# Dividing in two instructions per step in a fused DFT and two-layer kernel on one Trainium2 core

## What is computed

```python
X = np.fft.fft(np.fft.fft(x, axis=1), axis=2).real      # x: (2, 3008, 256)
h = X.reshape(6016, 256) @ moe_w_in                     # 256 -> 2048
g = np.maximum(h, 0.0) ** 2
z = g @ moe_w_out                                       # 2048 -> 256
h = z @ moe2_w_in                                       # 256 -> 2048
P = a[0] + a[1] * h + a[2] * h**2 + a[3] * h**3
Q = 1.0 + abs(b[0]) * abs(h) + abs(b[1]) * h**2
out = (P / (Q + 1e-06)) @ moe2_w_out                    # 2048 -> 256
```

## Time and profile before

| what | value |
|---|---|
| median of 3 runs | 1017.86 us (1017.8 to 1018.49) |
| profiled execution | 1018.51 us, of which the span of instructions is 1016.7 us |
| granted TensorE clock, mean | 0.997 of full speed |
| busy share of PE, DVE, ACT, POOL | 98%, 93%, 89%, 58% |
| loop | from about 62 us to 940 us, then the drain |

### The profile page before, as it was taken

The page is one execution under the profiler, slowest core; times in us unless marked ns, Lnnn a source line. Parts: engine busy times, 40 slices in busy tenths (PEclk is TensorE's granted clock), DMA queues, the critical chain, the costliest instruction groups (busy, mean ns, idle before and its releaser), DMA issues.

```text
span 1016.7 us, 13778 instructions
## 1 busy us (share of the span) xinstructions
PE 993.7 (98%) x5112; PEld 846.1 (83%) x5112; DVE 948.2 (93%) x1039; ACT 906.2 (89%) x935; POOL 591.5 (58%) x316
## 2 busy tenths in 40 slices
PE   9999989999999999999999999999999999999987
PEld 8888878888888888888888888888888888888876
DVE  2668899999999999999999999999999999999998
ACT  2358899999999999999999999999999999999896
POOL 0358565655656556565565655656656565565475
PEclk9999999999999999999999999999999999999999
DMA  9885000001001001001001001001000000000000
GB/s 240 310 262 184 2 1 27 1 1 48 1 1 47 1 1 47 1 1 47 1 1 47 1 1 47 1 1 41 7 1 20 23 1 18 5 21 1 1 21 16
DMA packets 25918, 38.02 MB, mean 37 GB/s; under 512 B 1806, under 2 KB 19098, under 8 KB 25722
## 3 DMA queue, kind: packets, MB, share of 16 engines
q1 hardware_dynamic: 25804, 37.14, 11.7%
q10 hardware_dynamic: 48, 0.02, 0.0%
HBM read 25.31 MB, written 11.84 MB: 37 GB/s over the span
## 4 chain that ended last, share of the span: by engine, by line
PE 48%; DVE 40%; issue 9%; ACT 1%; DMA 1%; POOL 1%; SPq 0%; DVEq 0%; ACTq 0%; POOLq 0%
PE ps L963 25%; PE ps L954 12%; DVE den_s L801 6%; DVE den_s L812 6%; DVE den_s L814 5%; DVE g_value L802 5%; DVE g_value L822 5%; PE ps L979 3%; PE ps L991 3%; DVE g_value L794 3%; PE ps L895 3%; DVE g_value L795 3%; DVE ps L766 2%; PE ps L921 1%; DVE g_value L804 1%
## 5 line engine op out<-in xcount | busy, mean ns | idle before, releaser
L963 PE MATMUL ps<-g_hi,w_out_lo 128*128 128x512 f32 (+1 forms) x764 | 298.2, 390 | 5.5 <-POOL w_in_lo L551 3.1
L963 PE MATMUL ps<-g_hi,w_out_hi 128*128 128x512 f32 (+1 forms) x764 | 298.4, 391 | 0.0
L549 POOL CAST g_hi<-g_value 128x1024 fp32r<-128x1024 f32 x86 | 89.6, 1042 | 336.5 <-DVE g_value L822 336.5
L963 PE MATMUL ps<-g_lo,w_out_hi 128*128 128x512 f32 (+1 forms) x728 | 283.2, 389 | 0.0
L551 POOL TENSOR_TENSOR g_lo<-g_value,g_hi 128x1024 fp32r<-128x1024 f32 x86 | 208.2, 2421 | 6.9
L542 POOL TENSOR_TENSOR g_lo<-g_value,g_hi 128x1024 fp32r<-128x1024 f32 (+1 forms) x86 | 203.7, 2368 | 5.8 <-ACT g_hi L612 5.8
L963 PEld LDWEIGHTS ps<-g_hi,w_out_lo 128*128 128x128 f32 x764 | 144.6, 189 | 33.0 <-POOL w_in_lo L551 3.8
L963 PEld LDWEIGHTS ps<-g_hi,w_out_hi 128*128 128x128 f32 x764 | 144.0, 188 | 29.1
L963 PEld LDWEIGHTS ps<-g_lo,w_out_hi 128*128 128x128 f32 x728 | 137.5, 189 | 25.5
L954 PE MATMUL ps<-z_hi,w_in_lo 128*128 128x512 f32 x352 | 111.2, 397 | 5.9 <-DVE g_value L804 5.9
L812 DVE SCALAR_TENSOR_TENSOR den_s<-den_s,seed_s 128x1024 f32<-128x1024 f32 x86 | 115.9, 1347 | 0.3 <-ACT seed_s L656 0.3
(11 more groups left out here) (135 smaller groups left out, 1917.1 us busy)
## 6 DMA issues: line engine op xcount, KB each, us to landing
x_s<-x SPq DMA_DIRECT2D x15, 384.0 KB, 6.9
out_t<-out_s SPq DMA_DIRECT2D x11, 512.0 KB, 5.4
w_out_unsplit_lo<-w_out SPq DMA_DIRECT2D x2, 2048.0 KB, 14.4
tw_s<-twiddle SPq DMA_DIRECT2D x1, 3012.0 KB, 15.9
y_hi_dram<-y_stage_hi SPq DMA_DIRECT2D x10, 256.0 KB, 5.1
y_lo_dram<-y_stage_lo SPq DMA_DIRECT2D x10, 256.0 KB, 5.8
w_in_raw<-w_in SPq DMA_DIRECT2D x4, 512.0 KB, 8.1
w_in_unsplit_lo<-w_in SPq DMA_DIRECT2D x4, 512.0 KB, 6.7
```

Of the source, the lines that this page charges most:

```text
L963: last = nc.tensor.matmul(acc[:, mb, 0:n], w[a][:, f, mb * P:(mb + 1) * P], g[c][:, i, 0:n], start=(f == 0 and j == 0), stop=(f == FB - 1 ...
```

## The change

Three things are changed.

1. `divide` in the loop becomes `divide_by_halves`: two instructions on 128x512 instead of one on 128x1024, for each of 85 units. The first signals `g2_first_half`, the second `g2_done`.
2. `split2` in the loop becomes `split2_by_halves`: GpSimd casts the first half once `g2_first_half` is there, the second once `g2_done` is there, and then subtracts in one instruction as before.
3. For the 30 units in `HALVED` (from 7 on, those whose number modulo 8 is 7, 0 or 1), line 804 becomes two instructions of 128x512, the first of which signals `h2_first_read`. `up2(m)`, for a unit m-1 in that list, waits for the first half before its first bank and for the second before its second bank. For all other units it waits as before.

```diff
+HALVED = tuple(m for m in range(UNITS - 1, DRAIN - 1) if m % UNITS in (UNITS - 1, 0, 1))
...
+            def split2_by_halves(m):
+                g, hi, lo = num_of(m), hi2_of(m), lo2_of(m)
+                pool.wait_ge(g2_first_half, m + 1)
+                after(pool, prod2_done, m - 1)
+                nc.gpsimd.tensor_copy(hi[:, 0, :], g[:, 0, :])
+                pool.wait_ge(g2_done, m + 1)
+                nc.gpsimd.tensor_copy(hi[:, 1, :], g[:, 1, :]).then_inc(g2_hi, 1)
+                pool.wait_ge(g2_hi, m + 1)
+                nc.gpsimd.tensor_tensor(lo, g, hi.bitcast(F32), ALU.subtract).then_inc(g2_lo, 1)
...
             for s in range(HEAD, STEPS):
                 if s > SKEW:
-                    split2(s - SKEW - 1)
+                    split2_by_halves(s - SKEW - 1)
                 keep_lo1(s)
...
-                nc.vector.scalar_tensor_tensor(num, num, a1, h2, ALU.add, ALU.mult).then_inc(h2_read, 1)
+                if m in HALVED:
+                    for i, done in enumerate((h2_first_read, h2_read)):
+                        nc.vector.scalar_tensor_tensor(num[:, i, :], num[:, i, :], a1, h2[:, i, :], ALU.add, ALU.mult
+                                                       ).then_inc(done, 1)
+                else:
+                    nc.vector.scalar_tensor_tensor(num, num, a1, h2, ALU.add, ALU.mult).then_inc(h2_read, 1)
...
+            def divide_by_halves(m):
+                den, num = den_of(m), num_of(m)
+                dve.wait_ge(rec_done, m + 1)
+                dve.wait_ge(h2_read, m + 1)
+                for i, done in enumerate((g2_first_half, g2_done)):
+                    nc.vector.scalar_tensor_tensor(num[:, i, :], num[:, i, :], a0, den[:, i, :], ALU.add, ALU.mult
+                                                   ).then_inc(done, 1)
...
                 if before is not None:
                     reciprocal(before)
-                    divide(before)
+                    divide_by_halves(before)
...
             def up(h, w, src, m, n, ready):
 
                 for i in range(2):
+                    if i == 1 and m - 1 in HALVED:
+                        pe.wait_ge(h2_read, m)
...
                 elif m == 2:
                     pe.wait_ge(h2_read, 1)
+                elif m - 1 in HALVED:
+                    pe.wait_ge(h2_first_read, HALVED.index(m - 1) + 1)
                 elif m > 2:
                     pe.wait_ge(h2_read, m - 1 if m > DRAIN else m)
```

More of the change, by code:

```diff
@@ L248, in fft_moe_kernel @@
         q_signed, t_h_done, h2_read = sem("q_signed"), sem("t_h_done"), sem("h2_read")
+        h2_first_read = sem("h2_first_read")
         q_done, ln_done, seed_done = sem("q_done"), sem("ln_done"), sem("seed_done")
         t_done, rec_done, g2_done = sem("t_done"), sem("rec_done"), sem("g2_done")
+        g2_first_half = sem("g2_first_half")
         act_a0, pool_g2_done = sem("act_a0"), sem("pool_g2_done")
```

## The result

The changed kernel takes 1024.62 us (median of 6 runs, 1024.29 to 1024.96) against 1017.85 us: a ratio of 1.0067 with a 95% interval of 1.0056 to 1.0078, or 6.8 us more. The forecast was 1025.5. The profiled execution has a span of 1022.9 us, against 1016.7.

The account below looks back on a forecast made before the run. DVE, in a ring with GpSimd, was taken to set the pace; + 0.82 us a tile gave + 7.4 in nine tiles, plus 0.3 after, + 7.7 in all: 1025.5 us, 8-in-10 range 1019.5 to 1031.

Parts of the forecast that it names:

- a ring: Ordinary steps: division, GpSimd's cast and subtractions, held line 812, line 814, next division; 9.65 us a step.
- The price of a split: DVE's division and line 804, scalar from SBUF: each split costs 0.13 us, with 0.05 as the other end.
- Rival B: DVE and GpSimd: splits cost 0.05 to 0.07 us, GpSimd comes 0.19 us or more earlier; 1013 us, chance 0.04.
- the last case there: DVE and GpSimd: cheap split but casts held, + 0.2 us a tile; 1019.7 us, chance 0.05.
- The held cast: GpSimd's first half cast: held by the division's second half, ending 0.49 us after it, shown about 1.05 us long.
- The second cast: GpSimd's second half cast: ends 1.06 us after the division, against 1.11 for the whole cast now.
- The gain for the ring: GpSimd's casts in two: 0.05 us shorter in each of seven ordinary steps of a tile.
- Rival A: GpSimd's first cast isn't held and doesn't hold DVE; 1018.9 to 1020 us, chance 0.08.
- Rival C: GpSimd's cast takes the turn between the division's halves, 0.54 us an ordinary step; 1058 us, chance 0.03.
- The third part: Line 804 in two: costs nothing in two of three steps, 0.13 us in the long step.
- PE's wait: PE's 0.52 us wait for line 804 in the long step: goes, short ones spread elsewhere; worth nothing to the time.

Follow-up runs that it names:

- experiment 4: Kernel before with GpSimd's cast in two, both after the whole division, DVE's instructions unchanged: 1026.84 us, ratio 1.0083.
- experiment 1: Changed kernel with only the division in two; GpSimd's cast and line 804 whole again: 1029.18 us, ratio 1.0100 against the kernel before.
- experiment 5: Kernel before with half of GpSimd's cast left out from unit 2 to 84, old numbers kept there: 1017.75 us, ratio 0.9996.
- experiment 8: Kernel before with line 814 in two, its scalar in the instruction; division and casts whole: 1023.20 us, ratio 1.0050.
- experiment 2: Changed kernel with line 804 whole in all units, division and casts still in halves: 1024.39 us, ratio 1.0055 against the kernel before.
- experiment 3: Changed kernel with division and casts whole, only line 804 in two for three units a tile: 1019.83 us, ratio 1.0011 against the kernel before.
- experiment 7: Kernel before with half of GpSimd's cast left out and line 804 in two for three units a tile: 1016.14 us, ratio 0.9981.
- experiment 9: Kernel before with half of GpSimd's cast left out and line 804 in two for five units a tile: 1014.36 us, ratio 0.9956.

## Why the prediction was right, and where it wasn't

**DVE and GpSimd set the pace in a ring.** This is shown from both sides: 0.13 us more on GpSimd alone came out in the time (experiment 4), 0.13 us more on DVE alone too (experiment 1), and once GpSimd's part is cut DVE starts to wait for ScalarE (experiment 5). The tile was forecast at 78.9 us and is 78.75.

**The price of a split.** 0.13 us was forecast for the form with a scalar in SBUF: the halves take 1.33 us against 1.21, and experiment 1 gives 1.06 a tile, 0.13 a step. The cheap split of Rival B and of the last case there is real, but for the other form: 0.06 to 0.07 us in experiment 8. So the figure of the Trainium skill ("VectorE: DVE Perf Modes", the section on the TRN2 errata), some 0.06 us for each instruction, agrees with line 814 within 0.01 us, and is half of what the division's form costs.

**The held cast.** Forecast 0.49 us after the division, measured 0.48, and its row shows 1.07 us as said. The second cast ends 1.04 us after the division (532.87), forecast 1.06. The gain for the ring was put at 0.05 us in each of seven steps, 0.35 a tile. Experiments 1 and 2 differ in the casts alone, and there a tile falls from 79.14 to 78.60 us: 0.54, or 0.08 a step. This is the term that was mis-sized. The two others were right: the division in two costs 79.14 - 78.08 = 1.06 a tile (forecast 1.04), the third part 78.75 - 78.60 = 0.15 (forecast 0.13). So a tile grew by 0.67 us and not by 0.82, which makes 6.0 us in nine tiles and not 7.4. The other 0.8 of the measured 6.8 us lies outside these tiles, where 0.3 was forecast, or in the scatter of the times; no run separates the two. It made up for a part of the error, and the forecast came out 0.9 us too high.

**Rivals A and C.** The first cast was held in each step and never came between the halves of a division (1.33 us for both), so neither happened.

**The third part.** Costing it at nothing in two of three steps was right: experiment 3 gives + 1.1 us where three full splits would have given 3.5, and in its trace line 812 takes 1.28 us in those two steps, 0.13 less than the 1.41 before. What was wrong is what the trace would show. The step said that PE's wait goes from the long step. It didn't: the long step of PE is still 10.27 us. With 1.2 us a tile to spare PE arrives earlier: it starts the long step 501.23 - 500.17 = 1.06 us after the division, and 499.26 - 497.72 = 1.54 us before. So it stands for `keep_z_lo`, for which it had no wait before, and for the first half of line 804. What the halves do take away shows against experiment 2, where the long step is 10.75; it comes back three steps later, at the first whole reader, as one wait of 0.5 us and not as many short ones. None of this had a part in the sum.

**What was missed.** The prediction read that DVE never waits and took PE's wait as worth nothing. It is worth nothing only as long as the ring is there. Experiment 5 shows that the two limits were equal within 0.1 us a tile (78.08 for a tile before, against 9.69 x 7 + 10.19 = 78.02 with the ring open), and experiments 7 and 9 that both have to go for either to pay.

## What to carry to other kernels

An instruction split in two so that a partner on another engine can start earlier pays only if the partner gains more than the split costs. Here the partner couldn't run beside the second half: it came 0.08 us earlier, and the split cost 0.13. Look for instructions that get longer when another engine is at work: such a hold stands in no list of waits, and an engine that is busy for 58% can be on the path through it. When two limits are equally long, removing one gains nothing; take the other away by leaving work out before judging.

## What the runs showed of the hardware

- A held instruction is shown as a long one. A cast of 512 columns takes 0.61 to 0.62 us and is shown as 1.07 when DVE has two tensors in SBUF beside it; it ends 0.48 us after DVE does, 0.14 sooner than its own length, as if its start were done while it is held. Line 812 likewise ends 1.08 us after GpSimd, and takes 1.22 alone.
- The fixed part of a DVE instruction in a row of them depends on its form: 0.12 to 0.13 us for a scalar that is read from SBUF (1.33 us for two halves, 1.21 for the whole), 0.06 to 0.07 for one in the instruction (0.61 for a half, + 5.1 us for the kernel in experiment 8 against + 10).
- The Trainium skill, "SBUF — State Buffer", section "Who interferes with whom", calls the shared port pair an exclusive lock and says that the order of issue decides who blocks. The trace agrees: the second half of a division had started 0.16 us before the cast was let go, and the cast waited.
